# Block sums of the values on 32-column products in a fused attention and two-layer gated kernel (Trainium2, one core)

## What is computed

```python
k_sum = k.reshape(B, H, nb, 32, D).max(axis=3)
v_sum = v.reshape(B, H, nb, 32, D).mean(axis=3)      # the block sums of this case
scores_all = concat([where(|i-j|<16, scale*q@k.T, -1e9), scale*q@k_sum.T + log(32)])
a = exp(scores_all - max); a = a / (sum(a) + 1e-9)
x = a @ concat([v, v_sum])                           # 1536 x 512 over both batches
x = (silu(x @ w_gate) * (x @ w_val)) @ w_out         # 512 -> 1536 -> 512
h = x @ w_in                                         # 512 -> 2048
y = where(h <= -1, 0, where(h >= 1, h, (h+1)**2/4)) @ w_out2
```

## Time and profile before

| | |
|---|---|
| median of 3 runs | 609.03 us |
| the profiled execution, its own time | 608.4 us |
| its span in the profile | 606.3 us |
| PE busy | 97% |
| DVE / ACT / POOL busy | 77% / 60% / 14% |
| mean granted TensorE clock | 0.997 |
| chain that ended last | PE 82%, DVE 9%, ACT 5% |

### The profile page before, as it was taken

The page is one execution under the profiler, slowest core; times in us unless marked ns, Lnnn a source line. Parts: engine busy times, 40 slices in busy tenths (PEclk is TensorE's granted clock), DMA queues, the critical chain, the costliest instruction groups (busy, mean ns, idle before and its releaser), DMA issues.

```text
span 606.3 us, 10568 instructions
## 1 busy us (share of the span) xinstructions
PE 586.3 (97%) x3912; PEld 540.4 (89%) x3912; DVE 469.5 (77%) x906; ACT 363.2 (60%) x733; POOL 86.4 (14%) x80
## 2 busy tenths in 40 slices
PE   3989999999999999999999999999999999999997
PEld 3667789989899999999999999998878899998886
DVE  6789788988585667778776767998998479979833
ACT  4776888888755456666634545664655456655522
POOL 3760232432300002232210000000000000000000
PEclk9989999999999999999999999999999999999999
DMA  9985442442122112223212111321111323002212
GB/s 331 242 302 159 129 138 79 132 131 97 53 61 62 53 35 70 71 69 122 88 53 70 53 36 69 122 88 46 60 52 53 139 70 122 2 35 73 67 53 104
DMA packets 31330, 57.50 MB, mean 95 GB/s; under 512 B 3184, under 2 KB 5744, under 8 KB 31280
## 3 DMA queue, kind: packets, MB, share of 16 engines
q1 hardware_dynamic: 31120, 56.57, 28.8%
q10 hardware_dynamic: 160, 0.26, 0.2%
HBM read 52.23 MB, written 3.15 MB: 91 GB/s over the span
## 4 chain that ended last, share of the span: by engine, by line
PE 82%; DVE 9%; ACT 5%; issue 2%; DMA 1%; POOL 0%; ACTq 0%; POOLq 0%; SPq 0%; DVEq 0%
PE ps L589 45%; PE ps L726 18%; PE ps L698 15%; ACT prob_s L843 1%; DVE hid_lo L1231 1%; PE ps L557 1%; PE ps L579 1%; DMA k_raw<-k_t_dram 1%; PE ps L550 1%; DVE rel L1237 1%; PE ps L517 1%; DVE h L1240 1%; DVE x_lo L1163 1%; DVE wout_lo L1225 1%; ACT prob L843 1%
## 5 line engine op out<-in xcount | busy, mean ns | idle before, releaser
L589 PE MATMUL ps<-x_hi,w_hi 128*128 128x384 f32 x560 | 192.1, 343 | 1.3 <-DVE h L1219 0.4
L589 PE MATMUL ps<-x_lo,w_hi 128*128 128x384 f32 x560 | 187.4, 335 | 0.0
L589 PE MATMUL ps<-x_hi,w_lo 128*128 128x384 f32 x560 | 187.2, 334 | 0.0
L589 PEld LDWEIGHTS ps<-x_hi,w_hi 128*128 128x128 f32 x560 | 105.1, 188 | 6.0 <-issue 3.7
L589 PEld LDWEIGHTS ps<-x_hi,w_lo 128*128 128x128 f32 x560 | 105.2, 188 | 1.1 <-issue 1.0
L589 PEld LDWEIGHTS ps<-x_lo,w_hi 128*128 128x128 f32 x560 | 105.1, 188 | 0.0
L962 ACT ACTIVATE wout_hi<-wout_raw 128x512 fp32r<-128x512 f32 x56 | 35.3, 631 | 95.1 <-PE ps L726 52.0
L726 PE MATMUL ps<-wout_hi,hid_hi 128*128 128x512 f32 x192 | 74.8, 390 | 0.8 <-DVE wout_lo L1225 0.8
L726 PE MATMUL ps<-wout_hi,hid_lo 128*128 128x512 f32 x192 | 75.2, 392 | 0.1
L726 PE MATMUL ps<-wout_lo,hid_hi 128*128 128x512 f32 x192 | 74.8, 389 | 0.0
L1225 DVE TENSOR_TENSOR wout_lo<-wout_raw,wout_hi 128x512 fp32r<-128x512 f32 x56 | 39.4, 704 | 40.1 <-ACT wout_hi L962 39.6
(11 more groups left out here) (119 smaller groups left out, 925.6 us busy)
## 6 DMA issues: line engine op xcount, KB each, us to landing
w_raw<-w_dram SPq DMA_DIRECT2D x80, 256.0 KB, 2.9
wout_raw<-w_dram SPq DMA_DIRECT2D x56, 256.0 KB, 2.6
out_dram<-y_out SPq DMA_DIRECT2D x12, 256.0 KB, 2.1
v_s<-v_rows_dram SPq DMA_DIRECT2D x6, 384.0 KB, 11.9
v_a<-v_rows_dram SPq DMA_DIRECT2D x6, 384.0 KB, 3.7
v_tok_a<-v_rows_dram SPq DMA_DIRECT2D x3, 512.0 KB, 7.9
k_raw_b<-k_t_dram SPq DMA_DIRECT2D x3, 512.0 KB, 7.5
v_tok_b<-v_rows_dram SPq DMA_DIRECT2D x3, 512.0 KB, 9.4
```

The source lines that it names most:

```text
L589: last = nc.tensor.matmul(dst, lhs, rhs, start=start and kk == 0 and i == 0, stop=kk == 1 and i == 2, skip_group_check=not start)
```

## The change

- The sums of a batch become three groups of four products. A product takes 32 columns of `sel` (now 40 wide), all 128 rows of a chunk and 256 of its 512 columns. The four of a group go to four column strips of the array and of the bank: strip j holds half `j // 2` of the blocks and half `j % 2` of the value columns. Chunks i and i+3 are loaded together.
- Groups 0 and 1 of batch 0 go behind the scores of step 2, group 2 behind those of step 3, ahead of the transposes. DVE copies 128x256 at step 3 to `v_part`. Batch 1's groups stand behind `p1(0)`, `p6(0)` and `p5(0)`.
- The rows are put in place by DMA alone: four per group of tiles, issued by SP. Tiles 0 to 5 and 6 to 11 for batch 0 (eight DMAs), all four tiles of `v_a` for batch 1 (four DMAs, moved from ACT's queue to SP's, behind `load_late(7)`).
- The load order: `load_v(0)` to `load_v(2)` earlier, the first wait for the sums ahead of `load_q(4)`, `load_v(3)`, `load_q(5)`; `load_w(1)` behind `load_v(5)`.
- `denom`: the 1e-9 stands in a second column of `total`, and `tensor_reduce` adds the two.

```diff
-SEL0 = WIN + (VCH - 1) * (P // BLOCK)
+SEL0 = 2 * (P // BLOCK)
+VHALF = NB // 2
...
-SUMS_WITH = {3: (0, 1), 4: (2, 3), 5: (4, 5)}
-SUMS_AT = ((2, 4), (4, 8), (8, TILES))
+SUMS_WITH = {2: (0, 1), 3: (2,)}
+SUMS_AT = ((0, 6), (6, TILES))
...
             def load_v_tok(b):
-                for c in range(0, VCH, 2):
-                    sp.dma_start((v_tok_a, v_tok_b)[b][:, c:c + 2], src[:, c:c + 2]).then_inc(v_tok_loaded[b][c // 2], 16)
+                for c in range(VCH // 2):
+                    sp.dma_start((v_tok_a, v_tok_b)[b][:, c::VCH // 2], src[:, c::VCH // 2]).then_inc(v_tok_loaded[b][c], 16)
...
+            def place_sums(b, dst, ready):
+                for j in range(4):
+                    half, y = divmod(j, 2)
+                    n = P - WIN - VHALF if half else VHALF
+                    row = WIN + half * VHALF
+                    part_of = v_part[BLOCK * j:BLOCK * j + n, b].unsqueeze(1).to_broadcast([n, dst.shape[1], DM // 2])
+                    sp.dma_start(dst[row:row + n, :, y * (DM // 2):(y + 1) * (DM // 2)], part_of).then_inc(ready, 16)
...
-                sp.dma_start(v_s[WIN:, c0:c1], v_sum[WIN:, 0].unsqueeze(1).to_broadcast([P - WIN, c1 - c0, DM])
-                             ).then_inc(v_first_sums[j], 16)
+                place_sums(0, v_s[:, c0:c1], v_first_sums[j])
+
+            def place_late_sums():
+                sp.wait_ge(v_sum_ready, 2)
+                sp.wait_ge(trans_done, LAST_A)
+                place_sums(1, v_a[:], v_late_sums)
...
             load_q(2)
+            load_v(0)
+            load_v(1)
             load_q(3)
-            load_v(0)
+            load_v(2)
+            place_first_sums(0)
             load_q(4)
-            load_v(1)
+            load_v(3)
             load_q(5)
-            load_v(2)
-            load_w(1)
-            load_v(3)
-            place_first_sums(0)
             place_first_sums(1)
-            place_first_sums(2)
             load_v(4)
             load_v(5)
+            load_w(1)
...
             load_late(7)
+            place_late_sums()
             load_w(4)
...
-                if i % 2 == 0:
-                    pe.wait_ge(v_tok_loaded[b][i // 2], 16)
-                c0 = SEL0 - WIN - i * (P // BLOCK)
-                last = nc.tensor.matmul(v_sum_ps[b][:], sel[:, c0:c0 + P], (v_tok_a, v_tok_b)[b][:, i],
-                                        start=i == 0, stop=i == VCH - 1)
+                pe.wait_ge(v_tok_loaded[b][i], 16)
+                c0 = SEL0 - i * (P // BLOCK)
+                for j in range(4):
+                    half, y = divmod(j, 2)
+                    last = nc.tensor.matmul(v_sum_ps[b][BLOCK * j:BLOCK * j + BLOCK, 0:DM // 2], sel[:, c0:c0 + BLOCK],
+                                            (v_tok_a, v_tok_b)[b][:, half * (VCH // 2) + i, y * (DM // 2):(y + 1) * (DM // 2)],
+                                            start=i == 0, stop=i == VCH // 2 - 1)
...
-                    if s == 0:
-                        pe.wait_ge(v_pair_sums, 1)
-                    for j, (c0, _) in enumerate(SUMS_AT):
-                        if s == c0:
-                            pe.wait_ge(v_first_sums[j], 16)
-                    if pr in (FIRST, FIRST + 1):
-                        pe.wait_ge(v_late_sums[pr % 2], 16)
+                    for j, (first, _) in enumerate(SUMS_AT):
+                        if s == first:
+                            pe.wait_ge(v_first_sums[j], 64)
+                    if pr == FIRST:
+                        pe.wait_ge(v_late_sums, 64)
...
                 first_scores(s)
+                for i in SUMS_WITH.get(s, ()):
+                    value_sums(0, i)
...
-                for i in SUMS_WITH.get(s, ()):
-                    value_sums(0, i)
...
+            p1(0)
             value_sums(1, 0)
-            value_sums(1, 1)
-            p1(0)
             p2(0)
-            value_sums(1, 2)
-            value_sums(1, 3)
...
-                        value_sums(1, 4)
+                        value_sums(1, 1)
...
-                        value_sums(1, 5)
+                        value_sums(1, 2)
...
-                nc.scalar.activation(v_sum[WIN:, b], v_sum_ps[b][WIN:, :], ACT.Copy).then_inc(v_sum_ready, 1)
-
-            def place_late_sums(j):
-                act.wait_ge(v_sum_ready, 2)
-                act.wait_ge(trans_done, LAST_A)
-                act.dma_start(v_a[WIN:, 2 * j:2 * j + 2], v_sum[WIN:, 1].unsqueeze(1).to_broadcast([P - WIN, 2, DM])
-                              ).then_inc(v_late_sums[j], 16)
+                nc.scalar.activation(v_part[:, b], v_sum_ps[b][:, 0:DM // 2], ACT.Copy).then_inc(v_sum_ready, 1)
...
-                        place_late_sums(0)
-                        place_late_sums(1)
...
-            def place_v_sum():
+            def copy_first_sums():
                 dve.wait_ge(v_sum_done, 1)
-                nc.vector.tensor_copy(v_sum[WIN:, 0], v_sum_ps[0][WIN:, :]).then_inc(v_sum_ready, 1)
-                nc.vector.tensor_copy(v_s[WIN:, 0:2], v_sum_ps[0][WIN:, :].unsqueeze(1).to_broadcast([P - WIN, 2, DM])
-                                      ).then_inc(v_pair_sums, 1)
+                nc.vector.tensor_copy(v_part[:, 0], v_sum_ps[0][:, 0:DM // 2]).then_inc(v_sum_ready, 1)
...
-                nc.vector.tensor_scalar(denom[:, c], total[:, c], 1e-9, None, ALU.add).then_inc(denom_ready, 1)
+                nc.vector.tensor_reduce(denom[:, c], total[:, c], AX.X, ALU.add).then_inc(denom_ready, 1)
...
+            nc.vector.memset(total[:, :, :, 1:2], 1e-9)
...
-                if s == 5:
-                    place_v_sum()
+                if s == 3:
+                    copy_first_sums()
```

More of the change, by code:

```diff
@@ L153, in build @@
         k_a = at("k_a", 185344, [4, COLS // SUB, PAIRS, SUB])
-        v_sum = at("v_sum", 193536, [B, DM])
+        v_part = at("v_part", 193536, [B, DM // 2])
         masked = at("masked", 197632, [2, PAIRS, COLS])
-        sel = at("sel", 201728, [SEL0 - WIN + P])
+        sel = at("sel", 201728, [SEL0 + BLOCK])
         rel = at("rel", 203776, [2, S])
@@ L162, in build @@
         neg_max = at("neg_max", 212480, [RING, PAIRS])
[L163 to L166, removed]
+        total = at("total", 212544, [RING, PAIRS, 2])
+        denom = at("denom", 212672, [RING, PAIRS])
+        inv = at("inv", 212736, [RING, PAIRS])
+        half = at("half", 212800, [1])
         ps = ctx.enter_context(nc.psum_tensor("ps", [P, 8, 512], F32))
@@ L252, in build @@
         v_first_loaded = [sem(f"v_first_loaded{j}") for j in range(FIRST)]
-        v_pair_sums = sem("v_pair_sums")
         v_first_sums = [sem(f"v_first_sums{j}") for j in range(len(SUMS_AT))]
         v_late_loaded = [sem(f"v_late_loaded{j}") for j in range(2)]
-        v_late_sums = [sem(f"v_late_sums{j}") for j in range(2)]
+        v_late_sums = sem("v_late_sums")
         scores_done = sem("scores_done")
@@ L513, in value_sums @@
                         pe.wait_ge(masked_ready, LAST_A - 1)
-                if i % 2 == 0:
-                    pe.wait_ge(v_tok_loaded[b][i // 2], 16)
-                c0 = SEL0 - WIN - i * (P // BLOCK)
-                last = nc.tensor.matmul(v_sum_ps[b][:], sel[:, c0:c0 + P], (v_tok_a, v_tok_b)[b][:, i],
-                                        start=i == 0, stop=i == VCH - 1)
-                if i == VCH - 1:
+                pe.wait_ge(v_tok_loaded[b][i], 16)
[5 more added lines that the diff above has]
+                                            start=i == 0, stop=i == VCH // 2 - 1)
+                if i == VCH // 2 - 1:
                     last.then_inc(v_sum_done, 1)
@@ L843, in exponentials @@
                     last = nc.scalar.activation(prob_of(s)[:, a], masked[:, s % 2, a], ACT.Exp, scale=-1.0,
-                                                bias=neg_max[:, c, a:a + 1], accum_out=total[:, c, a:a + 1])
+                                                bias=neg_max[:, c, a:a + 1], accum_out=total[:, c, a, 0:1])
                 last.then_inc(exp_done, 1)
```

## The result

Twelve executions of each kernel in turns: the changed kernel takes 612.08 us in the median (609.46 to 615.18), the one before 610.15 (608.56 to 611.82). The ratio is 1.0039, 95% interval 1.0023 to 1.0055: slower by 2.4 us, where 4.0 us less were forecast. The profiled execution took 610.47 us (span 608.7), one of the shorter ones.

A forecast was written before the change was run, and what follows sets the result against it. PE bounds from 76.17 us on; ahead of it PE, DVE and ACT take turns, so only that start can move. 3.7 + 0.5 - 0.1 - 0.1 = 4.0 us gained: median 605.0 instead of 609.03, range 603.8 to 608.6.

The forecast's parts named there:

- Part 1: Sums of batch 0 on PE: a group of four takes 0.6 us, so 1.8 us instead of 5.5.
- Part 2: First twelve steps: ACT back to back ends at 34.7 instead of 38.5, the others keep up; gain 3.7 us.
- Part 3: `denom` on DVE: at most 0.2 us each; only the last counts on the chain, gain taken as 0.5 us.
- Part 4: Batch 0's rows placed by SP's DMAs: values 0 late by 0 to 0.3 us, 0.1 taken; later loads cost nothing.
- Part 5: Batch 1: PE's saving worth nothing beyond DVE's shift; placed rows late by 0 to 1.4 us, 0.1 taken.
- part of the gain is eaten by a wait or the clock: Rows late for step 7 or 12, or PE's clock falling: gain only 1.8 to 3 us, say 606.6; 24%.
- Two of the other rivals: Four products of a group don't overlap, 611 us, 6%; PE's clock falls again and again, 611 us, 3%.

The follow-up runs named there:

- run 13: Kernel of run 5 with all queries loaded first, then value rows, `load_w(1)` and batch 1 each behind a step's scores: 606.13 us, 0.9947 to the kernel before.
- run 5: Changed kernel without the eight placing DMAs of batch 0, whose block values are left out: 610.84 us, 1.0010 to the kernel before.
- run 7: Changed kernel with six groups of four products on 128 columns, first two tiles filled by DVE, three placing DMAs of whole rows: 612.23 us, 1.0031.
- run 18: Changed kernel, halves and eight placing DMAs kept, with loads paced behind steps' scores and most of batch 1 behind step 12's: 613.13 us, 1.0050.
- run 9: Kernel of run 5 with SP waiting for six steps' scores ahead of `load_w(1)` and eight steps' ahead of batch 1's loads: 610.74 us, 1.0021.
- run 12: Kernel of run 5 with SP waiting for eight steps' scores ahead of batch 1's keys alone: 610.82 us, 1.0016.
- run 14: Kernel of run 7 with all queries loaded first and the other loads paced behind steps' scores: 608.86 us, 0.9989.
- run 17: Kernel of run 14 with `load_k_raw(1, 0)` behind step 8's scores and the rest of batch 1's loads behind step 12's: 608.62 us, 0.9980.
- run 4: Kernel before with `load_w(1)` moved behind `load_v(5)` and nothing else: 610.43 us, 1.0002.
- run 16: Kernel before with all queries loaded first and other loads paced behind steps' scores, its sums and three placing DMAs kept: 612.50 us, 1.0043.
- run 1: Changed kernel with `load_w(1)` moved behind `load_v(2)`, ahead of SP's wait for the sums: 616.93 us, 1.0106 to the kernel before.
- run 2: Changed kernel with `load_w(1)` moved behind `load_v(3)`: 613.64 us, 1.0038 to the kernel before.
- run 10: Changed kernel with SP waiting for six steps' scores ahead of `load_w(1)` and eight steps' ahead of batch 1's loads: 613.25 us, 1.0057.
- run 11: Kernel of run 7 with SP waiting for six steps' scores ahead of `load_w(1)` and eight steps' ahead of batch 1's loads: 611.77 us, 1.0040.

## Why the prediction was wrong

**Part 1 right.** A group of four took 0.57 to 0.59 us, forecast 0.6; neither 0.76 nor 1.82. The late groups took 0.64 with their start.

**Part 2 right about ACT's pace, wrong that others keep up.** ACT was back to back to 24.0 us and then lost 1.78 and 2.23 us to waits for PE. That the gain was there to be had is shown by run 13: 3.3 us less than the kernel before, against 4.0 forecast, with batch 0's placing left out.

**Part 3 right.** `denom` is 0.16 us. Alone it gave 0.13% (0.28% to -0.01%), 0.8 us where 0.5 was taken; that isn't told apart from nothing.

**Part 4 is the step that failed**: "SP [...] issues nothing from about 8.2 to 16.4, and the queue empties. So I take 3 to 4 us to landing, and no loss." Three terms of it were mis-sized, and a fourth was put at nothing.
1. The queues don't empty. Their share is 0.94 to 1.06 in the stretches between 10 and 46 us, and still 1.03 from 16.50 to 17.00, when the first placing DMA is issued, 8 us behind the last load. A row that the prediction had in hand, 0.97 over 10.95 to 38.56, spoke against an empty queue. Query 3, issued at 7.24, came late for 20.60 (1.03 us).
2. An issue was taken as 0.69 us; the eight took 7.57, 0.95 each, 2.05 us more in all.
3. Landing: the first four were issued by 20.01 and values 0 began at 24.59, 4.6 us later; taken were 2.5 to 4.1 from the start of an issue. That the placing is what they wait for is shown by runs 5 and 7, where the wait is gone, and by run 18, where it is 5.01 behind other loads. `load_w(1)` took 8.47 us to land and not 3 to 4.
4. Left out altogether: PE's instructions come through the same DMA engines. The kernel before issued its loads up to 12.64, then let SP wait until 23.47 for the sums; its sums also kept PE behind its instructions: it was through its 449th instruction at 22.66 us, where the changed kernel was at 17.41. Take the sums away, and PE reaches the end of its supply while the queues are full.

The evidence for the fourth is the place and the time of the stops. The place first. In run 9 PE stops at 18.55, 28.89 and 35.64, and between these stops stand as many records of PE and its weight load each time (125 and 125, 126 and 125; columns as in the earlier trace rows):

```profile
18.54:28.88 10.34, 7.99 (x125) 6.62 (x125) 4.39 (x31) 8.21 (x36) 7.00 (x8) 0.67 1.06 271
28.88:35.63 6.75, 5.22 (x126) 4.34 (x125) 3.75 (x22) 4.69 (x19) 4.82 (x4) 1.00 1.01 387
```

With the waits for semaphores, which this view leaves out, the packed trace has exactly 256 in either stretch. Every stop of 0.4 us or more in the middle of a group up to 45 us, in the changed kernel and in all runs, stands behind the 449th, the 705th or the 961st of these records, 256 apart, whatever the products around it are. So it is not an operand that is late there.

The time: each of those in the table ends 2.5 to 2.8 us behind the start of a 16 KB packet of the instruction queue q8. For runs 5, 9, 12 and 13, which have the same program on PE, it has the stop behind record 705:

| run | behind record | stop, us | packet between | PE goes on |
|---|---|---|---|---|
| 5 | 705 | 4.12 | 26.50 and 26.75 | 29.30 |
| 9 | 705 | 1.25 | 26.00 and 26.25 | 28.89 |
| 12 | 705 | 1.10 | 25.25 and 25.50 | 28.00 |
| 13 | 705 | 2.38 | 24.25 and 24.50 | 27.03 |
| 7 | 961 | 2.83 | 31.50 and 31.75 | 34.23 |
| 14 | 961 | 4.72 | 30.50 and 30.75 | 33.37 |
| 17 | 961 | 1.83 | 27.00 and 27.25 | 29.51 |
| changed | 449 | 1.04 | 15.75 and 16.00 | 18.68 |

The packet itself is short, a third of 16 engines over 0.25 us, 1.3 us of one engine; what varies is when it comes. That the loads set this is shown by the same four runs, whose kernels differ in SP's list alone: PE was through record 449 at 17.5 to 18.0 us in all of them, and the next packet started at 26.7, 26.3, 25.3 and 24.3. In runs 4 and 16, the kernel before with its sums, the queues were nearly empty over 22 to 26 us (DMA share 0.09 and 0.02), and there the packet came 1.5 and 1.4 us ahead of PE's record 449, where run 5 had it 9.1 us behind. In the kernel before the packets stand at 14.75, 23.0, 29.25 and 35.5, and PE has no such stop. The Trainium skill ("Runtime: NRT & Kernel Launch", Instruction fetch mechanics) has each sequencer fetch its program in blocks of 16 KiB, 256 instructions, through a DMA queue of its own, and calls the cost mostly hidden. The trace agrees on the block: the stops are 256 records apart, the 8,121 records of PE and its weight load (waits included) are 31.7 blocks, and q8 has 31 packets; run 7 has 8,218 records, 32.1 blocks, and 32 packets. It doesn't agree on "hidden" while the loads fill the queues: up to 4.7 us a time here.

**Part 5.** The late rows came 0.76 us late (67.62); forecast 0 to 1.4, taken 0.1. PE's idle time ahead of `p6(0)` was 0.54 us, not 2, since PE itself came late.

**The rival that came true** is the first one, "part of the gain is eaten by a wait or the clock", in a size it wasn't given (its lowest gain was 1.8). Its places are the right ones but one: rows for step 7, rows for step 12, the clock. The clock was 0.59 in 39.3 to 42.8 and 0.50 over 42 to 46, behind 3.24 us without work, where the kernel before had 0.52 and 0.90. The forecast took these as single prices. In runs 1, 2 and 9 to 12 a wait that was taken away or shortened was followed by another wait or by a stretch at the lower clock, and no time was gained. Two of the other rivals had times near the measured one, 611, but by mechanisms that the trace rules out: the groups overlapped (0.57 to 0.59), and the clock didn't fall before 38 us (1.00 in every stretch from 10 to 38).

**Sum.** Of the 6.4 us between forecast (4.0 less) and result (2.4 more), the placing carries some 1.8 (run 5 against the changed kernel, 0.29%), the order and pacing of the loads 3.8 (run 13 against run 5, 0.63%), each with 1.2 to 1.3 of uncertainty; the 0.8 that are left are less than that. The two aren't additive in general: taken alone, pacing left the changed kernel where it was (run 18).

**What stays open.** The profile shows no request of an instruction block, only its packet, so how long one waits behind the loads is known only against the place that PE had reached. The length of a stop is no measure of it, since it depends on when PE arrives as well: run 13 has 2.38 us with the earliest packet of the four, where PE came there at 24.65, and run 9 has 1.25, where PE came at 27.64. How much of the 3.8 us is instructions and how much query 3 and the other loads wasn't parted by a run. Whether a complete version can have run 13's time wasn't settled: run 17 is the best found, 0.9980, not told apart from the kernel before.

## What to carry to other kernels

When work is taken off PE at the start of a kernel, ask what it hid: how full the DMA queues are, which small transfers and which instruction blocks must pass through them, and when. Count small SBUF-to-SBUF copies by their number, of packets in a full queue and of issues on the engine that issues them, and issue bulk loads no earlier than needed where PE is what waits; in the kernel before, which had no such stops, the same pacing lost 2.6 us. A gap of PE that is closed may open the next one or lower the clock behind it, so judge such a change by whole runs, and by the stretch in which the limiting engine is back to back.

## What was not expected of the hardware

- PE stopped in the middle of a row of products that wait for nothing, for 0.6 to 4.7 us, always at a multiple of 256 records from the same place, and went on 2.5 to 2.8 us behind the start of a packet of its instruction queue (table above).
- Half rows of 1 KB took as long in the queues as packets of 2 KB: 120 ns for 1,024 bytes at 20 to 22 us in the changed kernel, 109 ns for 2,048 bytes at 18 to 22 us in the one before; the rates there were 135 and 318 GB/s. The Trainium skill ("DMA: Bandwidth & Descriptors", Why small descriptors are slow (HBM only)) has copies within SBUF free of a penalty for small pieces; the packets of 20 to 22 us don't bear that out beside other loads.
- An issue of a placing DMA took 0.69 us in the kernel before and 0.77 to 1.58 in the changed one.
- A reduce of eight elements took 158 ns where a `tensor_scalar` of four took 408 beside a busy POOL.
